# The result's way out of a token and channel mixing kernel: VectorE 32x32 transposes and small stores in place of TensorE transposes, token down begun on half of h1, a second bank for early attention values

## The chip, the cores and the metric

The kernel runs on one core of one Trainium2 chip. The metric is the device time of one execution in microseconds; the median of several executions counts, lower is better. All matrix work is fp32 in quality: most products are made from two fp32r parts of each operand (hi and lo), three matmuls for each product.

## The reference

Three stages, batch B = 4, sequence S = 576, model width DM = 512.

```python
attn = softmax(mask(q @ k.T / 8)) @ v      # 8 heads of 64; window 32, for heads 4 to 7 dilated by 4
x = attn as [B, S, 512]
# feed forward with token shift
xk = mu_k * x + (1 - mu_k) * x_prev;  xr = mu_r * x + (1 - mu_r) * x_prev
x = sigmoid(xr @ w_r) * (relu(xk @ w_k) ** 2 @ w_v)              # w_k 512x1024, w_v 1024x512
# token and channel mixing
h = relu(x.T @ w_tok1) @ w_tok2            # 576 -> 256 -> 576 over the tokens
u = x + h.T
out = u + relu(u @ w_ch1) @ w_ch2          # 512 -> 1536 -> 512
```

## The kernel before, in words

The program has no loops at run time. Each stage is a list of steps, and a step is a small set of functions, one for each engine that takes part; every engine's instruction stream is its functions in the order of the list. Engines meet at semaphores only, so the order of the list is the order on each engine's queue, and a waiting instruction holds all that is behind it on its engine.

Phase 1 holds attention and the feed-forward stage. Attention works in 24 groups n (12 blocks of 192 tokens, each for the plain heads and for the dilated ones). The first four groups run in a prologue whose list is written out by hand (`prologue`): transposes of q and k into the two halves of the PSUM tensor `tq2`, scores into `s2`, softmax over VectorE, GpSimd and ScalarE, transposes of p, then `weighted_values(n)` (L605) into the bank `o_ps`, from which `x_evict(n)` (L621) copies into X on ScalarE. `weighted_values(n)` waits until group n - 1's copy is done, since there is one such bank. `keep_warm` steps put idle matmuls between. Behind the copy of group 3 the feed-forward stage begins: `difference` (L645, GpSimd, its subtraction L651), `mix` (L654, VectorE, L664), and the first products of `up` (L744). From then on attention groups 4 to 23 are strewn between the feed-forward units. X holds the transposed activations (features on partitions, tokens along the row).

Phase 2 (`phase2_body`) takes one batch b after the other:

- `x_transpose` (L971) transposes the batch's activations `xcur` (loaded by a GpSimd request, `load_x` L936) into rows, and splits them; these steps of batch b + 1 are in the list of batch b, between the last channel-up tile and the last two channel-down tiles.
- `token_up` (L1006), two tiles m of 128x512 of h1: 15 matmuls each (5 token tiles x 3), then Relu into the high part on ScalarE (L1025) and the low part on VectorE (L1029).
- `out_transpose` (L1144), five tiles of 120 (the last 96) tokens: four TensorE transposes each of U into one of the four work banks (L1153), a ScalarE copy into an `ost` buffer (L1159), and one store of up to 120 rows of 2 KB by SyncE (L1163).
- `token_down` (L1032), eight tiles (half h of the tokens, feature tile d): 6 matmuls each, and U = product + xcur on VectorE (L1050). In batch 0 alone the four tiles of the first half are made by `first_token_down` (L1053), which starts on the first 128 rows of h1 and needs the second later.
- `token_parts` (L1069) splits u; `channel_up` (L1084) makes 24 tiles of 12 matmuls, each with a Relu (L1103) and a low part (L1107); `channel_down` (L1110) follows two tiles behind and adds into four accumulators `acc[d]`, 12 matmuls for each f (L1131 to L1133), with one signal `c2_done` at the end of the four.
- `finish` (L1135) adds the four accumulators into U on VectorE (L1141), once for each half h, after the last channel-down of the half.

Products with two parts go through `product` (L686), whose three matmuls are L694, L695 and L696. The four work banks (`bank[0]`, `bank[1]`, the halves of `tq2`) are used in turn in the order of the table `ORDER`: 8 token-down tiles, 24 channel-up tiles, 5 of x, 2 of token-up, 5 output tiles, 44 in all, a multiple of 4. `work_free` makes TensorE wait until the user four places earlier has been read. The list of a batch ends like this:

```python
            return steps + ups + [out_transpose(b, tt) for tt in range(NTT)]
```

so TensorE's order at a batch boundary is: token up of the next batch, the 20 transposes of this batch's result, token down of the next.

## Time and profile before

| | us |
|---|---|
| median of 3 executions | 768.98 (768.02 to 769.06) |
| the profiled execution | 766.38 |
| its span on the core | 764.5 |
| TensorE matmuls busy | 737.9 (97%) |
| VectorE busy | 354.7 (46%) |
| ScalarE busy | 257.3 (34%) |
| GpSimd busy | 221.2 (29%) |

The span runs from the first to the last recorded instruction of the profiled execution; the execution's own time is 1.9 us longer. Matmuls overlap: a matmul of 128x288 is shown with some 0.3 us, but the next one starts 0.13 us after it. So the distance between starts is the cost in a row of matmuls, and the shown duration counts only where something waits for the last one. A bracket at the end of a timeline row gives the idle time of the engine before the row and who ended it.

### The profile page before, as it was taken

The numbers are of one execution on the slowest core, as the hardware profiler recorded it, in microseconds if no ns is written. First come the engines' busy times: TensorE is split into PE (matmuls) and PEld (weight loads), VectorE is DVE, ScalarE is ACT, GpSimd is POOL, SyncE is SP. The second block draws the span as 40 slices with busy tenths as digits, with TensorE's granted clock in tenths as the row PEclk, the third lists the DMA queues.
The fourth block names the chain that finished last, engine by engine and source line by source line (L and its number), as shares of the span: only waits on it lengthen the run. The fifth ranks groups of instructions, "written<-read, shape, count | busy, mean of one in ns | idle before, by whom it ended". The sixth has DMA issues, their size and how long they took to land.

```text
span 764.5 us, 15730 instructions
## 1 busy us (share of the span) xinstructions
PE 737.9 (97%) x6650; PEld 712.8 (93%) x6650; DVE 354.7 (46%) x590; ACT 257.3 (34%) x641; POOL 221.2 (29%) x237
## 2 busy tenths in 40 slices
PE   7889899999999999999999999999999999999997
PEld 7778899898998989899989999999999999999997
DVE  6488756676575757666661213412134121341211
ACT  4565453535345353525351112411124111241112
POOL 5395664546456464636018000000000000000000
PEclk9999999999999999999999999999999999999999
DMA  9922132120230230020641000300003000020002
GB/s 199 289 50 66 22 78 59 28 61 23 55 75 21 52 76 19 1 63 1 235 158 42 21 1 1 124 3 1 1 1 124 1 1 1 1 63 1 2 1 63
DMA packets 67942, 39.82 MB, mean 52 GB/s; under 512 B 55264, under 2 KB 59168, under 8 KB 67872
## 3 DMA queue, kind: packets, MB, share of 16 engines
q1 hardware_dynamic: 62559, 33.30, 17.0%
q0 software_dynamic: 1088, 4.72, 1.8%
q10 hardware_dynamic: 4224, 0.79, 0.7%
q8 instruction: 53, 0.87, 0.5%
q14 instruction: 18, 0.14, 0.1%
HBM read 29.36 MB, written 4.72 MB: 45 GB/s over the span
## 4 chain that ended last, share of the span: by engine, by line
PE 84%; POOL 6%; issue 3%; ACT 3%; DVE 3%; ACTq 1%; DVEq 0%; POOLq 0%
PE bank L694 14%; PE bank L695 13%; PE bank L696 13%; PE tq L694 5%; PE tq L696 5%; PE tq L695 5%; PE s L1133 3%; PE bank L1133 3%; PE bank L1132 3%; PE bank L1131 3%; PE s L1131 3%; PE s L1132 3%; PE bank L615 3%; PE bank L587 2%; PE s L497 2%
## 5 line engine op out<-in xcount | busy, mean ns | idle before, releaser
L694 PE MATMUL bank<-k_hi,WV_hi 128*128 128x288 f32 x256 | 79.1, 309 | 0.0
L694 PE MATMUL bank<-xk_hi,WK_hi 128*128 128x288 f32 x224 | 69.5, 310 | 9.6 <-DVE kr L757 8.4
L695 PE MATMUL bank<-k_hi,WV_lo 128*128 128x288 f32 x256 | 76.3, 298 | 0.0
L696 PE MATMUL bank<-k_lo,WV_hi 128*128 128x288 f32 x256 | 76.0, 297 | 0.0
L1107 DVE SCALAR_TENSOR_TENSOR h_lo<-tq,h_hi 128x288 fp32r<-128x288 f32 x48 | 22.0, 458 | 115.9 <-ACT h_hi L1103 115.9
L1107 DVE SCALAR_TENSOR_TENSOR h_lo<-bank,h_hi 128x288 fp32r<-128x288 f32 x48 | 22.0, 458 | 115.5 <-ACT h_hi L1103 115.5
L772 POOL TENSOR_TENSOR k_lo<-kr,k_hi 128x288 fp32r<-128x288 f32 x64 | 53.4, 836 | 71.8 <-ACT k_hi L768 71.5
L695 PE MATMUL bank<-xk_hi,WK_lo 128*128 128x288 f32 x224 | 66.2, 296 | 0.0
L696 PE MATMUL bank<-xk_lo,WK_hi 128*128 128x288 f32 x224 | 66.0, 294 | 0.0
L805 DVE RECIPROCAL rg<-rg 128x288 f32<-128x288 f32 x32 | 62.5, 1953 | 1.1
L1103 ACT ACTIVATE h_hi<-tq 128x288 fp32r<-128x288 f32 x48 | 19.7, 411 | 127.2 <-PE tq L696 127.2
L1103 ACT ACTIVATE h_hi<-bank 128x288 fp32r<-128x288 f32 x48 | 19.7, 410 | 117.8 <-PE bank L696 117.8
L1133 PE MATMUL s<-h_lo,C_hi 128*128 128x288 f32 x192 | 57.0, 297 | 0.0
L1133 PE MATMUL bank<-h_lo,C_hi 128*128 128x288 f32 x192 | 57.0, 297 | 0.0
L1132 PE MATMUL bank<-h_hi,C_lo 128*128 128x288 f32 x192 | 56.9, 297 | 0.0
L941 POOL DMA_DIRECT2D xcur<-X x4 | 3.2, 798 | 185.8 <-DVE U L1050 168.6
L1131 PE MATMUL s<-h_hi,C_hi 128*128 128x288 f32 x192 | 56.9, 297 | 0.0
L1131 PE MATMUL bank<-h_hi,C_hi 128*128 128x288 f32 x192 | 56.9, 296 | 0.0
L1132 PE MATMUL s<-h_hi,C_lo 128*128 128x288 f32 x192 | 56.7, 295 | 0.0
L694 PE MATMUL bank<-u_hi,C_hi 128*128 128x288 f32 x192 | 56.7, 295 | 0.0
L694 PE MATMUL tq<-u_hi,C_hi 128*128 128x288 f32 x192 | 56.7, 295 | 0.0
L695 PE MATMUL bank<-u_hi,C_lo 128*128 128x288 f32 x192 | 56.7, 295 | 0.0
(155 smaller groups left out, 2172.4 us busy)
## 6 DMA issues: line engine op xcount, KB each, us to landing
C_raw<-in_moe_w_ch SPq DMA_DIRECT2D x6, 1024.0 KB, 11.6
xcur<-X POOLq DMA_DIRECT2D x4, 1152.0 KB, 5.8
qraw<-in_q SPq DMA_DIRECT2D x20, 192.0 KB, 3.5
kraw<-in_k SPq DMA_DIRECT2D x20, 192.0 KB, 4.0
out_x<-ost SPq DMA_DIRECT2D x16, 240.0 KB, 2.7
vt<-in_v SPq DMA_DIRECT2D x40, 80.0 KB, 2.5
vt<-in_v SPq DMA_DIRECT2D x7, 320.0 KB, 3.3
WK_raw<-in_moe_w_k SPq DMA_DIRECT2D x4, 512.0 KB, 7.9
```

The source lines that it names most:

```text
L497: last = e.matmul(s2[64 * a:64 * a + 64, c0:c0 + KB], qT[rows, 256 * s + 64 * c:256 * s + 64 * (c + 1)], keys(rows, s, c), start=True, sto ...
L615: last = e.matmul(o_ps[64 * h:64 * h + 64, SU * s + QB * c:SU * s + QB * (c + 1)], raw_v(n, slice(0, KB), 2 * s + h)[:, D * c:D * (c + 1)] ...
L694: e.matmul(out_ap, wh, xh, start=start and i == 0, stop=False)
L695: e.matmul(out_ap, wl, xh, start=False, stop=False)
L696: last = e.matmul(out_ap, wh, xl, start=False, stop=stop and i == len(kts) - 1)
L772: e.tensor_tensor(lo, t, hi.bitcast(F32), ALU.subtract).then_inc(Z.lo_done, 1)
L805: e.reciprocal(t, t).then_inc(Z.r_done, 1)
L1103: e.activation(hi, ps, ACT.Relu).then_inc(Z.h2h_done, 1)
L1107: e.scalar_tensor_tensor(lo, ps, 0.0, hi.bitcast(F32), ALU.max, ALU.subtract).then_inc(Z.h2l_done, 1)
L1131: e.matmul(o_, wh, xh, start=f == 0, stop=False)
L1132: e.matmul(o_, wl, xh, start=False, stop=False)
L1133: return e.matmul(o_, wh, xl, start=False, stop=f == FT2 - 1)
```

## The change

It has five parts.

1. *Result of the batches.* The `out_transpose` steps are gone. `finish` is now four steps, one for each feature tile d, each waiting for its own tile's last matmul only; for that, `channel_down` signals `c2_done` after each of the four tiles (four times for each f), and waits on it count by four. `out_blocks(b, h, d)` transposes the 128x288 piece of U on VectorE in blocks of 32x32 into `blocks[h]`. For the first half of the tokens (h = 0) these steps stand in the channel loop of the second half, behind channel-down tiles 1 to 4; for h = 1 (batches 0 to 2) they stand behind the last `finish`, ahead of token up. `store(b, h)` issues 16 requests on SyncE, for each d and each group of 32 partitions one: 288 pieces of 32 values (128 bytes) each.
2. *Last half of the last batch.* `last_transposes(d)` makes three TensorE transposes of 96 tokens as soon as feature tile d is finished; `last_rows(g)` copies two feature tiles at a time (ScalarE two thirds, VectorE one third) and SyncE stores them in one request of 288 pieces of 1 KB.
3. *Token down.* `first_token_down` now serves every batch. h1's second tile gets its low part in two pieces of 256 columns, each with its own signal, and token down waits for the first piece before the feature tiles 0 and 1 of kt = 1 and for the second before tile 2.
4. *Work banks.* The output tiles are no longer in `ORDER`: 39 users for a batch, so the bank of a user now depends on the batch too.
5. *Early values.* Groups 1 and 3 of attention put their values into the upper half of `tq2` in place of `o_ps`; so groups 1, 2 and 3 wait for the copy of the group two before. The transposes of group 4's keys, which use the same half, wait for the copy of group 3.

The core of the diff:

```diff
-        ost = [at(f"ost{i}", [P, DM], F32, 4 * DM * i) for i in range(4)] + [at("ost4", [P, DM], F32, o)]
-        assert NTT == 5 and 4 * DM <= XB
-        o += 4 * DM
+        blocks = [at(f"blocks{h}", [P, DT * HALF], F32, 4 * DT * HALF * h) for h in range(2)]
+        rows3 = at("rows3", [P, 3 * DM], F32, -(-4 * XB // 64) * 64)
...
+                    if n == 4 and g == 1:
+                        e.wait_ge(Z.x_done, 4)
...
+        def o_bank(n):
+
+            return tq2[:, 512:1024] if n in (1, 3) else o_ps
...
             def tensor(e):
                 e.wait_ge(Z.ptb_done, n + 1)
                 e.wait_ge(*v_landed(n))
-                wait(e, Z.x_done, n)
+                if n in (1, 3):
+                    e.wait_ge(Z.k_done, 4)
+                wait(e, Z.x_done, n - 1 if n in (1, 2, 3) else n)
...
-                [("x", i) for i in range(NTT)] + [("t1", i) for i in range(2)] + [("ot", i) for i in range(NTT)]
+                [("x", i) for i in range(NTT)] + [("t1", i) for i in range(2)]
         TB = len(ORDER)
-        READ = {"x": (Z.xtl_done, NTT, 1), "t1": (Z.h1l_done, 2, 1), "t2": (Z.u_done, 8, 0), "c1": (Z.h2l_done, 2 * FT2, 0),
-                "ot": (Z.os_done, NTT, 0)}
-        assert TB % 4 == 0
-
-        def work_bank(kind, i):
-            return work[ORDER.index((kind, i)) % 4]
+        READ = {"x": (Z.xtl_done, NTT, 1), "t1": (Z.h1l_done, 3, 1), "t2": (Z.u_done, 8, 0), "c1": (Z.h2l_done, 2 * FT2, 0)}
+
+        def work_bank(b, kind, i):
+            return work[(TB * b + ORDER.index((kind, i))) % 4]
...
+            pieces = [(0, DM)] if m == 0 else [(0, DM // 2), (DM // 2, DM)]
+
+            def part(t, c):
+                return t[:, DM * m + c[0]:DM * m + c[1]]
...
-            def vector(e):
-                e.wait_ge(Z.h1h_done, n + 1)
-                e.scalar_tensor_tensor(lo, ps[:, :], 0.0, hi.bitcast(F32), ALU.max, ALU.subtract).then_inc(Z.h1l_done, 1)
+                e.activation(part(h1[0], (0, DM)), ps[:, :], ACT.Relu).then_inc(Z.h1h_done, 1)
+
+            def vector(e):
+                e.wait_ge(Z.h1h_done, 2 * b + m + 1)
+                for c in pieces:
+                    e.scalar_tensor_tensor(part(h1[1], c), ps[:, c[0]:c[1]], 0.0, part(h1[0], c).bitcast(F32), ALU.max,
+                                           ALU.subtract).then_inc(Z.h1l_done, 1)
...
-        def first_token_down():
-
-            def tensor(e):
-                e.wait_ge(Z.x2_done, DT * NU)
-                e.wait_ge(Z.h1l_done, 1)
+            return dict(tensor=tensor, vector=vector) if h else dict(vector=vector)
+
+        def first_token_down(b):
+
+            def tensor(e):
+                if b == 0:
+                    e.wait_ge(Z.x2_done, DT * NU)
+                e.wait_ge(Z.h1l_done, 3 * b + 1)
                 for d, kt in ((0, 0), (1, 0), (2, 0), (0, 1), (1, 1), (2, 1), (3, 0), (3, 1)):
                     if kt == 0:
-                        work_free(e, 0, "t2", d)
-                    elif d == 0:
-                        e.wait_ge(Z.h1l_done, 2)
-                    last = product(e, work_bank("t2", d)[:, 0:HALF], h1, cols(DM, P * d, P), T2, cols(S, 0, HALF), [kt],
+                        work_free(e, b, "t2", d)
+                    elif d in (0, 2):
+                        e.wait_ge(Z.h1l_done, 3 * b + (3 if d else 2))
+                    last = product(e, work_bank(b, "t2", d)[:, 0:HALF], h1, cols(DM, P * d, P), T2, cols(S, 0, HALF), [kt],
                                    start=kt == 0, stop=kt == 1)
                     if kt == 1:
                         last.then_inc(Z.t2p_done, 1)
...
-                    e.wait_ge(Z.c2_done, n - NH2 + 1)
+                    e.wait_ge(Z.c2_done, DT * (n - NH2 + 1))
...
-                    last = channel_product(e, d, f, i % NH2)
-                last.then_inc(Z.c2_done, 1)
+                    channel_product(e, d, f, i % NH2).then_inc(Z.c2_done, 1)
...
-        def finish(b, h):
-            def vector(e):
-                e.wait_ge(Z.c2_done, 2 * FT2 * b + FT2 * (h + 1))
+        def finish(b, h, d):
+            c = slice(S * d + HALF * h, S * d + HALF * (h + 1))
+
+            def vector(e):
+                e.wait_ge(Z.c2_done, DT * (2 * FT2 * b + FT2 * (h + 1) - 1) + d + 1)
                 e.wait_ge(Z.uh_done, 8 * b + 8)
+                e.tensor_tensor(U[:, c], acc[d][:, 0:HALF], U[:, c], ALU.add).then_inc(Z.fin_done, 1)
+            return dict(vector=vector)
+
+        out_done = (Z.out_done0, Z.out_done1)
+        OUT = 16 * 4 * DT
+
+        def out_blocks(b, h, d):
+
+            def vector(e):
+                e.wait_ge(Z.fin_done, 8 * b + 4 * h + d + 1)
+                if d == 0:
+                    wait(e, out_done[h], OUT * b)
+                e.transpose(blocks[h][:, HALF * d:HALF * (d + 1)], U[:, S * d + HALF * h:S * d + HALF * (h + 1)])\
+                    .then_inc(Z.ob_done, 1)
+            return dict(vector=vector)
+
+        def store(b, h):
+
+            def sync(e):
                 for d in range(DT):
-                    c = slice(S * d + HALF * h, S * d + HALF * (h + 1))
-                    e.tensor_tensor(U[:, c], acc[d][:, 0:HALF], U[:, c], ALU.add).then_inc(Z.fin_done, 1)
-            return dict(vector=vector)
-
-        def out_transpose(b, tt):
-            n = NTT * b + tt
-            nt = rows_of(tt)
-            ps = work_bank("ot", tt)
-
-            def tensor(e):
-                work_free(e, b, "ot", tt)
-                e.wait_ge(Z.fin_done, 8 * b + (4 if TT * tt + nt <= HALF else 8))
-                for d in range(DT):
-                    last = e.transpose(ps[0:nt, P * d:P * (d + 1)], U[:, S * d + TT * tt:S * d + TT * tt + nt], ident[:, :])
-                last.then_inc(Z.otp_done, 1)
-
-            def scalar(e):
-                e.wait_ge(Z.otp_done, NTT * b + tt + 1)
-                e.wait_ge(Z.ost_free, b + 1)
-                e.activation(ost[tt][0:nt, :], ps[0:nt, :], ACT.Copy).then_inc(Z.os_done, 1)
+                    e.wait_ge(Z.ob_done, 8 * b + 4 * h + d + 1)
+                    for g in range(4):
+                        c0 = P * d + 32 * g
+                        e.dma_start(out[b, HALF * h:HALF * (h + 1), c0:c0 + 32].rearrange("(c i) n -> i c n", i=32),
+                                    blocks[h][32 * g:32 * (g + 1), HALF * d:HALF * (d + 1)].rearrange("p (c n) -> p c n", n=32))\
+                            .then_inc(out_done[h], 16)
+            return dict(sync=sync)
+
+        TL = HALF // 3
+
+        def last_transposes(d):
+
+            def tensor(e):
+                if d == 0:
+                    e.wait_ge(Z.h2l_done, 2 * FT2 * B)
+                e.wait_ge(Z.fin_done, 8 * B - DT + d + 1)
+                for t in range(3):
+                    c0 = 2 * P * (t % 2) + P * (d % 2)
+                    last = e.transpose(work[2 * (d // 2) + t // 2][0:TL, c0:c0 + P],
+                                       U[:, S * d + HALF + TL * t:S * d + HALF + TL * (t + 1)], ident[:, :])
+                last.then_inc(Z.lt_done, 1)
+            return dict(tensor=tensor)
+
+        def last_rows(g):
+
+            dst = tiles(rows3[0:TL, :], 3)[:, :, 2 * P * g:2 * P * (g + 1)]
+
+            def scalar(e):
+                e.wait_ge(Z.lt_done, 2 * g + 2)
+                e.activation(dst[:, 0:2], tiles(work[2 * g][0:TL, :], 2), ACT.Copy).then_inc(Z.ra_done, 1)
+
+            def vector(e):
+                e.wait_ge(Z.lt_done, 2 * g + 2)
+                e.tensor_copy(dst[:, 2], work[2 * g + 1][0:TL, 0:2 * P]).then_inc(Z.rv_done, 1)
 
             def sync(e):
-                e.wait_ge(Z.os_done, n + 1 + NTT)
-                e.dma_start(out[bass.ds(b, 1), TT * tt:TT * tt + nt, :].rearrange("b t n -> (b t) n"), ost[tt][0:nt, :])\
-                    .then_inc(Z.out_done, 16)
-                if tt == NTT - 1:
-                    e.wait_ge(Z.out_done, 16 * (n + 1))
-                    e.sem_inc(Z.ost_free, 1)
-            return dict(tensor=tensor, scalar=scalar, sync=sync)
+                e.wait_ge(Z.ra_done, g + 1)
+                e.wait_ge(Z.rv_done, g + 1)
+                e.dma_start(out[B - 1, HALF:S, 2 * P * g:2 * P * (g + 1)].rearrange("(t p) n -> p t n", p=TL), dst)\
+                    .then_inc(out_done[1], 16)
+            return dict(scalar=scalar, vector=vector, sync=sync)
...
-                    if seq[i - 2][1] == FT2 - 1:
-                        steps.append(finish(b, seq[i - 2][0]))
-            return steps + ups + [out_transpose(b, tt) for tt in range(NTT)]
+                    h, f = seq[i - 2]
+                    if h == 1 and 1 <= f <= DT:
+                        steps.append(out_blocks(b, 0, f - 1))
+                    if f < FT2 - 1:
+                        continue
+                    steps += [finish(b, h, d) for d in range(DT)]
+                    if h == 1 and not last:
+                        steps += [out_blocks(b, 1, d) for d in range(DT)]
+            if last:
+                return steps + [store(b, 0)] + [last_transposes(d) for d in range(DT)] + [last_rows(g) for g in range(2)]
+            return steps + [store(b, 0), store(b, 1)] + ups + [first_token_down(nxt)]
```

## Rows read from the trace of the kernel before

**Rows 1.** The page, part 1: busy time, share of the span, instructions.

```profile
PE 737.9 (97%) x6650; PEld 712.8 (93%) x6650; DVE 354.7 (46%) x590; ACT 257.3 (34%) x641; POOL 221.2 (29%) x237
```

**Rows 2.** Windows: length, then PE, PEld, DVE, ACT, POOL busy; granted clock, DMA share, GB/s.

```profile
82.00:84.00 2.00, 2.00 (x10) 2.00 (x9) 1.97 (x4) 0.88 (x3) 1.06 (x2) 0.50 0.03 8
84.00:86.00 2.00, 2.00 (x35) 1.73 (x36) 0.55 (x2) 0.76 (x2) 1.21 (x1) 0.74 0.00 0
...
400.00:500.00 100.00, 99.80 (x736) 98.05 (x735) 26.14 (x58) 20.63 (x46) 18.04 (x10) 1.00 0.12 36
```

**Rows 3.** Timeline at the end of batch 0: start, duration, engine, line, what.

```profile
475.93 0.81 DVE L1141 TENSOR_TENSOR U<-bank,U 128x288 f32<-128x288 f32 x2
...
481.62 0.40 PE L696 MATMUL tq<-xT_lo,T_hi 96*128 96x512 f32 x1
481.86 0.60 PE L1153 MATMUL tq<-ident,U 128*120 128x128 f32 x4
...
482.69 0.69 DVE L1029 SCALAR_TENSOR_TENSOR h_lo<-tq,h_hi 128x512 fp32r<-128x512 f32 x1 [2.73 <-ACT h_hi L1025]
...
484.28 0.38 PE L694 MATMUL bank<-T_hi,h_hi 128*128 128x288 f32 x1
484.49 0.30 PE L695 MATMUL bank<-T_hi,h_lo 128*128 128x288 f32 x1
```

**Rows 4.** Timeline of TensorE in token down and in channel up of batch 1.

```profile
484.76 0.29 PE L694 MATMUL bank<-T_hi,h_hi 128*128 128x288 f32 x1
...
490.72 0.30 PE L694 MATMUL bank<-u_hi,C_hi 128*128 128x288 f32 x1
...
497.08 0.29 PE L694 MATMUL tq<-u_hi,C_hi 128*128 128x288 f32 x1
...
498.53 0.29 PE L696 MATMUL tq<-u_lo,C_hi 128*128 128x288 f32 x1
```

**Rows 5.** Timeline of batch 0's first token down.

```profile
390.31 0.40 PE L694 MATMUL bank<-T_hi,h_hi 128*128 128x288 f32 x1 [0.22 <-DVE h_lo L1029]
...
392.07 0.82 DVE L1050 TENSOR_TENSOR U<-bank,xcur 128x288 f32<-128x288 f32 x2 [1.82 <-DMA xcur<-X]
...
392.59 0.40 PE L694 MATMUL bank<-T_hi,h_hi 128*128 128x288 f32 x1
```

**Rows 6.** Timeline of the end of the program.

```profile
757.34 0.82 DVE L1141 TENSOR_TENSOR U<-s,U 128x288 f32<-128x288 f32 x2 [3.89 <-PE bank L1133]
...
759.04 0.62 PE L1153 MATMUL bank<-ident,U 128*120 128x128 f32 x4 [0.86 <-DVE U L1141]
...
760.67 0.59 ACT L1159 ACTIVATE ost<-tq 96x512 f32<-96x512 f32 x1
760.81 0.80 SPq L1163 DMA_DIRECT2D out_x<-ost  x2
```

**Rows 7.** Timeline of the prologue's end, attention groups 2 and 3.

```profile
28.38 1.14 PE L615 MATMUL bank<-pT,X 80*64 80x48 f32 x32 [0.73 <-ACT X L632]
...
29.55 0.88 ACT L632 ACTIVATE X<-bank 128x192 f32<-128x192 f32 x2 [1.32 <-PE bank L615]
...
30.51 1.29 POOL L651 TENSOR_TENSOR dif<-X 128x288 f32<-128x288 f32 x2 [0.91 <-ACT X L632]
...
32.17 1.24 PE L744 MATMUL bank<-x,WK_raw 128*128 128x288 f32 x4 [0.59 <-DVE x L664]
```

**Rows 8.** Costliest groups on VectorE of shape 128x288: busy, mean ns, idle before.

```profile
L805 DVE RECIPROCAL rg<-rg 128x288 f32<-128x288 f32 x32 | 62.5, 1953 | 1.1
...
L1141 DVE TENSOR_TENSOR U<-s,U 128x288 f32<-128x288 f32 x16 | 6.6, 454 | 11.3 <-PE bank L1133 11.3
```

**Rows 9.** Requests: size and landing; issue times on SyncE in ns; two in a timeline.

```profile
out_x<-ost SPq DMA_DIRECT2D x16, 240.0 KB, 2.7
...
L429 SPq DMA_DIRECT2D X<-in_v x8: 432/443/447, 10.8 to 14.2; - x8
...
18.78 6.24 SPq L365 DMA_DIRECT2D kraw<-in_k  x2
```

More of the change, by code:

```diff
@@ L961, in work_free @@
                 b, before = b - 1, before + TB
[L962 to L963 removed]
             k, n = ORDER[before]
             s, per, ahead = READ[k]
[L966 removed]
+            n = 2 * n if k == "t1" else n
+            wait(e, s, per * (b + ahead) + n + 1)
         def rows_of(tt):
```

34 lines of the change are left out of this document (12 added, 22 removed).

## The prediction

> **What bounds the kernel now.** I read the page's busy times first, then the windows by stage, then the timeline where the stages meet, at the start and at the end. TensorE is busy 97% of the span [rows 1]; in a stretch of the last stage it is busy 99.8 of 100 us at full granted clock, with VectorE and ScalarE at a quarter or less [rows 2]. There, work taken off TensorE shortens the time one for one, and work put on VectorE costs nothing until TensorE comes to wait for it. The timeline at the end of batch 0 shows what stands between two batches: the last token-up matmul of the next batch, twenty transposes of the result (20 more at each of the two later boundaries, placed the same), and only then token down [rows 3]. At the end and in the prologue TensorE isn't the limit, so there I follow the chain.
>
> **Boundaries, three times.** The transposes begin at 481.86 and token down at 484.28: 2.42 us, and the first matmul after them takes 0.21 us to the next one instead of 0.13 [rows 3]; so 0.08 more for a restart. After the change the nine matmuls that need only the first half of h1 begin at 481.86 and last 9 x 0.13 = 1.19, to 483.05. The tenth needs the low part of the second half. VectorE starts it at 482.69 and takes 0.69 for 512 columns; it is now cut in two. From 0.69 for 512 and 0.45 for 288 [rows 3, 8] a straight line gives 0.42 for 256, so the first piece ends at 483.11 and TensorE goes on at about 483.15: a wait of 0.10 and a restart of 0.08. The second piece ends by 483.5 and its reader starts at 483.9. Gain per boundary 2.42 + 0.08 - 0.10 - 0.08 = 2.32, three times 7.0. Bounds 2.1 (the cut pieces each as slow as a 288-column operation and a late start) to 2.5 (no wait at all): 6.3 to 7.5.
>
> **VectorE's transposes** aren't in the trace. Eight of 128x288 come to each of the three batches, four in the last. Four stand among the channel loop, where VectorE works a quarter of the time, and are free at any price below some 2 us (24 matmuls at 0.13, 3.2 us, for each of them). The other four stand at the boundary, after the final additions, which end at about 475.93 + 0.81 = 476.7 today, and ahead of h1's low parts. The first low part must be there at 481.86, and takes 0.69: so 481.1 - 476.7 = 4.4 us are free, 1.1 each; more, as the additions now start tile by tile. The nearest row is an addition of the same shape at 0.45; the far bound is the reciprocal at 1.95 [rows 8]. I take 0.45, which costs nothing. Below it nothing can be gained either: cover.
>
> **Signals.** channel_down now signals after each of its four tiles, 3 x 96 = 288 signals more. Token down has eight signals among the 45 intervals from 484.76 to 490.72, 0.1324 each; channel up has none in the 11 from 497.08 to 498.53, 0.1318 each [rows 4]. The difference over 45 intervals is 0.03 us, for eight signals 4 ns each, within the reading's 0.01; with that at most 9 ns. I take 0, with up to 2.6 us in the range. The Trainium skill, "TensorE: Matmul & The Clock Gate", section "The cost: per-tile semaphore tail", says that increments on completions queue up at 26.3 ns each. By that figure the 288 would cost an estimated 7.6 us and leave little of the gain; it is fitted on packed tiles, and no run here shows it.
>
> **First token down (batch 0).** It already starts on half of h1. The cut piece would end 0.27 earlier at the wait before 390.31; but the matmul at 392.59 waits for an addition that waits for xcur's transfer (1.82 us, to 392.07) [rows 5], and that transfer does not move. Gain 0.
>
> **The end.** Today the four additions start together at 757.34, the transposes that need them at 759.04, the last copy runs 760.67 to 761.26, the last store is issued right behind it and the span ends at 764.50 [rows 6]: 3.24 after the copy. After: each tile's addition starts when its own three matmuls are done; the first three hide under the last matmuls, the fourth runs 757.34 to 757.79. Twelve transposes of 96 rows at 0.12 (2.42 for twenty [rows 3]) run from about 757.1, one interval behind the last matmul; the last three start at 758.2, their result is there at 758.7 (two more and a last one of 0.3), the copy of 512 columns ends at 759.4 (0.59 and a step of 0.05). Plus 3.24 is 762.6. The last store carries 288 KB instead of 192; 240 KB land in 2.7 us [rows 9], less than the 3.24 for a larger one than today's last, so bytes are the small part and I add an estimated 0.3: 762.9, gain 1.6. If all of the 3.24 grew with the bytes, the gain would be 0.3; if nothing did and the copies of the two halves ran quicker, 2.5. The four VectorE transposes and sixteen stores of the first half start about 30 us before the end and lie under the channel loop.
>
> **Prologue.** Group 3's values wait 0.73 us for the copy of group 2's out of the same bank; then come the copy, the differences, the mixing and the matmul at 32.17 [rows 7]. With a second bank this chain moves up by 0.73; GpSimd has by then finished the two differences before it. Group 1's bank saves nothing: its matmuls waited for p, not for the bank. The new wait on group 3's keys and the transposes of group 4 are long met. I take 0.7. Bounds: 0, if GpSimd's queue, which the chain runs through from 37 us on, gives it back; and 1.5 more or less from the clock. That is because after two waits near 80 us the granted clock stood at 0.50 (the 1.2 GHz level) for 2 us and at 0.74 for 2 more [rows 2]: 1.0 + 0.5 lost, which another alignment may save or double.
>
> **Stores.** Each batch issues 32 requests of 288 pieces of 128 bytes in place of 5. SyncE takes 0.44 us for a small load request; the worst pair in the trace took 6.24 for two, with much in flight [rows 9]. Only SyncE is behind them; 32 x 0.44 = 14 us against a batch of 95. Cost 0.
>
> **Sum.** 7.0 + 1.6 + 0.7 = 9.3 on a span of 764.5, whose execution took 766.38: to 757.1. The median shown is 768.98, 2.6 above that execution, and the change touches nothing that explains the 2.6; so 759.7.
>
> **The rivals.**
> 1. *Signals cost.* With 9 ns each 2.6 us, 762.3; within my range. Only against [rows 4] could it be more: the signals would have to cost more in channel_down than they do in token down, and at three times the 9 ns the gain would still not be gone (767.5). Chance 0.06, of which 0.02 for more than 9 ns.
> 2. *VectorE becomes late at the boundary.* Transposes at the reciprocal's 1.95: the additions end about 475.6, then 7.8 us, so h1's first low part ends at 484.1 and token down starts there, as today. The 7.0 goes, 766.6 remains. Against it: of the costliest groups on VectorE with this shape only the reciprocal is above 0.5. The price begins to count between 1.1 and 1.4 each. Chance 0.04.
> 3. *The stores back up (slower).* The last batch's first half can be stored from about 719.3 on (19 groups of twelve matmuls at 0.1324 before 757.1 is 727, less the 7.7 gained by then), sixteen requests; the result's last stores stand behind them on SyncE. With t each, they hold the end from 719.3 + 16t + 3.2 > 755, t > 2.0, and make it slower than before from t > 2.6. At the worst pair's 3.12 the span ends at 772.4, the median is at 777. For it: pieces of 128 bytes. Against it: 0.44 for small requests in a row [rows 9]. The Trainium skill, "DMA: Bandwidth & Descriptors", section "Specifications", says that transfers under 512 B are read, modified and written; no run here has such a store. Chance 0.04.
> 4. *The bank and the tail give nothing, or the clock falls once more*: 7.0 - 1.5 + 0.5 = 6.0 or so, 763.0. Chance 0.08.
>
> **Chances.** Forecast 0.78, the four rivals 0.22. The forecast's own low end, with the clock's 1.5 back or a tail of 2.5 with boundaries of 2.5, is some 2.7 below: 757.0. The high end is 763.0 and holds rival 4 and rival 1 up to 9 ns; rivals 2 and 3 and the rest of 1 stay out. A measurement of this kernel can tell 0.2%, 1.5 us, from no change. All but rivals 2 and 3 are faster; rival 2 is faster by 0.3% at its price and nothing if dearer: same 0.03, slower 0.04, faster 0.93.
>
> **What would show it.** Right: at the boundary token down's matmuls directly behind token up's, with one wait of 0.1 to 0.2 for h1's low part; VectorE transposes of 0.3 to 0.6 us; matmul intervals of 0.13 in channel_down; group 3's values without a wait; 5 to 5.7 us from the last channel matmul to the end. Wrong: intervals above 0.14 behind channel_down's tiles (rival 1), TensorE waiting more than 1 us for h1 at the boundary (2), SyncE's store requests at over 2 us each (3), a second stretch at clock 0.5 (4).

## The result, and the profile after

| us | before | after |
|---|---|---|
| median beside each other, 4 executions each | 769.02 (768.02 to 772.4) | 761.85 (760.34 to 763.75) |
| the profiled execution | 766.38 | 763.75 |
| its span | 764.5 | 761.9 |
| first feed-forward matmul of the prologue starts at | 30.44 | 37.13 |
| from there to the first token-up matmul | 351.40 | 351.21 |
| first token-up matmul to the end of the span | 382.66 | 373.58 |

The ratio after to before is 0.990, interval 0.9861 to 0.994: 7.2 us less, where 9.3 was forecast. Executions of this kernel differ by some us, and the table's last three rows say where. The third stage repeats to within 0.5 us: 373.4 to 373.8 in the seven profiles in which it is as in the changed kernel, 382.5 to 382.9 in the four in which it is as before. The prologue doesn't repeat. So nearly every reading below splits the span at those two matmuls. The profiled pair differs by 2.6 only: 9.08 gained in the third stage, 0.19 in the middle, and 6.69 lost in the prologue. Two executions of a kernel below took 1014 and 1185 us, at a mean granted clock of 0.65 and 0.56; the ratios leave them out.

The page of the changed kernel; the first line answers to [rows 1], the store line to [rows 9]. The digits are the granted TensorE clock in 40 slices of 19 us.

```profile
PE 733.7 (96%) x6582; PEld 708.6 (93%) x6582; DVE 365.6 (48%) x624; ACT 248.5 (33%) x623; POOL 221.5 (29%) x237
...
PEclk8899999999999999999999999999999999999999
...
out_x<-blocks SPq DMA_DIRECT2D x112, 36.0 KB, 1.7
```

TensorE has 68 matmuls less: 80 transposes out, 12 in. VectorE has 11 us more and is no nearer its limit. The first two slices of the clock, 9 in the kernel before, are 8, so TensorE ran slower for part of the first 38 us.

**The boundary.** Timeline at the end of batch 0, where [rows 3] show the kernel before (bracket: idle time before the row and who ended it).

```profile
481.08 0.85 DVE L1148 TENSOR_TENSOR U<-bank,U 128x288 f32<-128x288 f32 x2
...
481.27 0.40 PE L703 MATMUL bank<-xT_hi,T_hi 120*128 120x512 f32 x1
...
481.85 1.54 DVE L1160 STREAM_TRANSPOSE blocks<-U 128x288 f32<-128x288 f32 x4
...
485.54 0.69 DVE L1038 SCALAR_TENSOR_TENSOR h_lo<-bank,h_hi 128x512 fp32r<-128x512 f32 x1 [2.15 <-ACT h_hi L1033]
...
487.90 0.40 PE L705 MATMUL tq<-xT_lo,T_hi 96*128 96x512 f32 x1
...
488.14 0.30 PE L703 MATMUL tq<-T_hi,h_hi 128*128 128x288 f32 x1
...
488.96 0.76 DVE L1038 SCALAR_TENSOR_TENSOR h_lo<-tq,h_hi 128x256 fp32r<-128x256 f32 x2 [2.74 <-ACT h_hi L1033]
...
489.20 0.29 PE L705 MATMUL bank<-T_lo,h_hi 128*128 128x288 f32 x1
...
489.45 0.40 PE L703 MATMUL tq<-T_hi,h_hi 128*128 128x288 f32 x1
...
494.71 0.30 PE L703 MATMUL tq<-u_hi,C_hi 128*128 128x288 f32 x1
```

The reader is to see three things. Token down follows token up after 0.24, one interval of a 512-column matmul (487.90, 488.14). Nine matmuls later the next starts 0.25 after its neighbour instead of 0.13: the one small wait, for h1's first low piece. And VectorE's four transposes take 1.54 together and end at 483.39; VectorE then idles 2.15 us until h1's first tile is there for its low part (485.54), so they delay nothing. SyncE's 16 requests start at 482.34 and take 9.79. From the first token-up matmul of a batch to its first channel-up it is 494.71 - 481.27 = 13.44 us; before it was 490.72 [rows 4] - 474.99 = 15.73. The row of the kernel before that this starts from:

```profile
474.99 0.40 PE L694 MATMUL bank<-xT_hi,T_hi 120*128 120x512 f32 x1
```

The later boundaries give 13.44 and 13.46 against 15.76 and 15.73.

**The end.** Timeline of the last us, against [rows 6].

```profile
755.30 0.86 DVE L1148 TENSOR_TENSOR U<-s,U 128x288 f32<-128x288 f32 x2 [2.66 <-PE s L1140]
...
756.12 0.86 DVE L1148 TENSOR_TENSOR U<-bank,U 128x288 f32<-128x288 f32 x2
756.18 0.30 PE L1140 MATMUL bank<-h_lo,C_hi 128*128 128x288 f32 x1
...
756.32 0.82 PE L1186 MATMUL bank<-ident,U 128*96 128x128 f32 x6
...
757.79 0.97 SPq L1206 DMA_DIRECT2D out_x<-rows  x2
...
757.83 0.59 ACT L1197 ACTIVATE rows<-tq 96x512 f32<-96x512 f32 x1
```

The additions now start while TensorE is still in the last channel matmuls, and the transposes follow at one interval. From the last channel matmul (756.18) to the end of the span (761.9) it is 5.72; before it was 7.49 (757.01 to 764.5). The last channel matmul of the kernel before:

```profile
757.01 0.30 PE L1133 MATMUL bank<-h_lo,C_hi 128*128 128x288 f32 x1
```

**VectorE's transposes and the stores**, grouped by the tile `blocks` (columns: duration in ns as least, median, most; first and last start).

```profile
L1171 SPq DMA_DIRECT2D out_x<-blocks x112: 315/455/1952, 450.1 to 738.5; - x112
L1160 DVE STREAM_TRANSPOSE blocks<-U x28: 434/467/469, 449.6 to 736.6; 128x288 f32<-128x288 f32 x28
...
DMA to landing us min/median/max: 1.5/1.7/3.3
```

**The start.** Timeline of the first 9 us of the changed kernel. SPq and ACTq are the requests issued by SyncE and ScalarE.

```profile
0.74 1.93 SPq L364 DMA_DIRECT2D qraw<-in_q  x4
...
4.32 1.78 ACTq L891 DMA_DIRECT2D mus<-in_moe_mu_k  x1
...
4.53 3.01 SPq L428 DMA_DIRECT2D vt<-in_v  x4
...
6.13 1.61 ACTq L891 DMA_DIRECT2D mus<-in_moe_mu_r  x1
...
7.85 0.49 ACT L466 ACTIVATE qT<-tq 128x384 f32<-128x384 f32 x1 [4.62 <-issue]
...
8.87 1.35 PE L498 MATMUL s<-kT,qT 64*64 64x80 f32 x32 [3.08 <-ACT kT L474]
```

The same stretch of the kernel before:

```profile
0.88 1.93 SPq L365 DMA_DIRECT2D qraw<-in_q  x4
...
4.53 4.08 SPq L429 DMA_DIRECT2D vt<-in_v  x4
...
5.62 1.28 ACTq L882 DMA_DIRECT2D mus<-in_moe_mu_r  x1
...
7.01 0.49 ACT L465 ACTIVATE qT<-tq 128x384 f32<-128x384 f32 x1 [3.83 <-issue]
...
8.03 0.78 PE L497 MATMUL s<-kT,qT 64*64 64x80 f32 x32 [1.50 <-ACT kT L473]
```

In the changed kernel SyncE's first request is 0.14 earlier, its `vt` requests are quicker, ScalarE's requests end at 7.74 instead of 6.90. ScalarE's first copy comes 0.84 later, TensorE waits 3.08 for it instead of 1.50, and the 32 score matmuls of the group, already at the lower clock, take 1.35 instead of 0.78. Windows of the changed kernel (length, busy time of PE, PEld, DVE, ACT, POOL, granted clock, DMA share, GB/s) show what follows:

```profile
8.00:12.00 4.00, 3.13 (x43) 2.99 (x44) 1.62 (x2) 1.49 (x4) 0.00 (x0) 0.53 1.39 175
12.00:16.00 4.00, 4.00 (x51) 3.61 (x51) 2.06 (x4) 1.24 (x3) 1.56 (x2) 0.61 1.07 295
...
24.00:28.00 4.00, 4.00 (x50) 3.72 (x52) 0.89 (x2) 2.22 (x7) 1.26 (x1) 0.67 1.04 221
28.00:32.00 4.00, 4.00 (x38) 3.88 (x35) 0.43 (x3) 1.54 (x5) 1.25 (x1) 0.50 1.17 274
```

The granted clock falls to 0.50, the 1.2 GHz level, at 8.3, while TensorE still waits, and comes back at 15.1. It falls again from 25.3 to 32.2, behind a wait of 1.74 us that ends at 23.95. The profile names this wait "issue": it shows nothing that TensorE waited for. In the kernel before all of 0 to 40 us ran at 1.00.

### The profile page after: what moved, and what is told of

It is laid out like the page before. It is cut to its first block, busy times and chain, and to the rows that moved or that the text cites. A ratio compares the mean times of both kernels' runs of the same rounds, so it can differ in the third digit from the quotient of the medians.

```text
span 761.9 us, 15692 instructions
## 1 busy us (share of the span) xinstructions
PE 733.7 (96%) x6582; PEld 708.6 (93%) x6582; DVE 365.6 (48%) x624; ACT 248.5 (33%) x623; POOL 221.5 (29%) x237
## 4 chain that ended last, share of the span: by engine, by line
PE 83%; POOL 6%; issue 3%; DVE 3%; ACT 2%; DMA 1%; ACTq 1%; DVEq 0%; POOLq 0%
PE bank L703 14%; PE bank L704 13%; PE bank L705 13%; PE tq L703 4%; PE tq L705 4%; PE tq L704 4%; PE bank L1140 3%; PE bank L1139 3%; PE s L1140 3%; PE bank L1138 3%; PE s L1138 3%; PE s L1139 3%; PE bank L624 3%; PE bank L588 2%; PE s L498 2%
## 5 line engine op out<-in xcount | busy, mean ns | idle before, releaser
L704 PE MATMUL tq<-u_hi,C_lo 128*128 128x288 f32 x192 | 56.6, 295 | 0.0
```

The lines of the kernel that those rows point to most:

```text
L704: e.matmul(out_ap, wl, xh, start=False, stop=False)
```

## The experiments

Where a ratio is given it is to the kernel before on the same chip, with its interval. "Third stage" is the stretch from the first token-up matmul to the end of the span, of the profiled execution.

### The changed kernel again, beside the next three

> The changed kernel itself, once more, as the yardstick for this chip. Theory: its gain from the first token-up matmul to the end is fixed by the schedule (9.1 us: three boundaries of 2.3 to 2.45 and 1.8 at the end), and what varies from run to run lies ahead of 45 us, where the granted clock falls to 0.50 after TensorE has waited for ScalarE's first two copies. So the ratio is 0.988 to 0.992, and the stretch from the first token-up matmul to the end of the span is within 0.2 us of 373.6 us. Rival (the small stores or the signals disturb TensorE now and then): that stretch itself varies by over 1 us.

761.83 (760.9 to 764.64, 10 executions) against 766.26 (29 executions): 0.9945, 0.9923 to 0.9967, which is outside the 0.988 to 0.992 expected. Third stage 373.58, to the hundredth the first profile's. First feed-forward matmul at 34.73, clock 0.50 for 3.4 us from 10.3 and from 24.0 again. With 29 executions of the kernel before, the gain is 4.4 us, not 7.2: the 769.0 of the first four was at the upper end of what that kernel does. The third stage gains 9.1, so something else loses some 4.7.

### One bank for early values

```diff
-            return tq2[:, 512:1024] if n in (1, 3) else o_ps
+            return o_ps
...
-                if n in (1, 3):
-                    e.wait_ge(Z.k_done, 4)
-                wait(e, Z.x_done, n - 1 if n in (1, 2, 3) else n)
+                wait(e, Z.x_done, n)
```

> The changed kernel with one bank for the early values, as before the change. Theory: group 3's value matmuls wait 0.7 us for group 2's copy again, and the first feed-forward matmul of tile 2 comes 0.7 us later behind group 2's copy; total plus 0.7 us against e1, if the clock in the prologue is the same in both. Rival (GpSimd's queue gives it back): the wait is back, but the distance from group 2's copy to GpSimd's first k_lo is within 0.2 us of e1's.

762.95, 0.9955 (0.9936 to 0.9973); first feed-forward matmul 35.11, with the same two falls of the clock. From the copy of group 2 to GpSimd's first `k_lo` it is 9.73 us with one bank (also in the kernel before) and 9.21 with two: the bank is worth 0.52 on that chain, not 0.73. GpSimd's four subtractions are next: with two banks they stand in a row without idle time and take 2.97 us (0.66 to 0.88 each, VectorE's mixing beside them), where with one bank the two pairs take 1.29 each. So the bank isn't what loses the 4.7; the prologue is as late without it.

### Token down waits for all of h1

```diff
-                e.wait_ge(Z.h1l_done, 3 * b + 1)
+                e.wait_ge(Z.h1l_done, 3 * b + 3 if b else 1)
```

> The changed kernel, but in batches 1 to 3 token down waits for all of h1's low parts before its first matmul. Theory: token down starts 1.7 us later at each of three boundaries (from 488.14 to 489.8 in the changed kernel's trace), less the wait of 0.12 and its restart that it has now: plus 1.4 to 1.6 each, plus 4.5 us in all against e1; that much of the 7.3 us from the boundaries would not have come by moving the transposes alone. Rival (VectorE's late parts could be covered otherwise): plus under 2 us.

767.69, 1.0005 (0.9977 to 1.0033), 13 executions. Third stage 377.79, so 4.21 longer. The waits of TensorE in it (total, times, longest):

```profile
PE tq L703 <- DVE h_lo L1038: 3.0, 2, 1.5
PE bank L703 <- DVE h_lo L1038: 1.5, 1, 1.5
```

One wait of 1.5 at each of three boundaries: half of h1 is worth 1.4 of the 2.3 gained at each. Taking the transposes from TensorE alone would have left 0.9, since h1's low part, hidden under them before, would be waited for.

The prologue of this profile tells something by chance. It is the lowest of the 13 executions (761.49): the clock fell once, for 3.4 us from 8.7, within a wait of 2.9, there was no "issue" wait behind 20 us, and the first feed-forward matmul starts at 30.66, 21.8 behind the first scores. Where the clock didn't fall at all (`mu` requested by GpSimd, below) it is 20.7, in the changed kernel's two profiles 28.3 and 25.6. So the first fall alone costs 1.1 us here; most of the cost is the "issue" wait and the fall behind it.

### Signals of every tile, in the kernel before

```diff
-                    last = channel_product(e, d, f, i % NH2)
-                last.then_inc(Z.c2_done, 1)
+                    channel_product(e, d, f, i % NH2).then_inc(Z.c2_done, 1)
```

with the two waits multiplied by four.

> The kernel before with one part of the change: channel_down signals after each of its four tiles, 288 signals more, and the waits count by four. Theory: nothing, within 0.3 us, in the stretch from the first token-up matmul to the end, and intervals of 0.13 us behind every tile. Rival (completion signals queue up, 26 ns each by the Trainium skill's page on TensorE, an estimate of 7.6 us): plus 7 us. By the upper bound of the reading, 9 ns each, plus 2.6 us.

765.89, 1.0003 (0.9986 to 1.002). Third stage 382.46 against 382.66: 288 signals more cost nothing that shows, less than 2 ns each by the 0.5 us to which the stage repeats. The Trainium skill, "TensorE: Matmul & The Clock Gate", section "The cost: per-tile semaphore tail", gives 26.3 ns for each; by that the stretch would be an estimated 7.6 us longer. Here, with signals 3 matmuls of 288 columns apart, the trace doesn't agree: nothing of the 7.6 shows. The tail it speaks of, increments of packed tiles at the end of a burst, wasn't tried.

### One signal for four tiles, in the changed kernel

```diff
-                    channel_product(e, d, f, i % NH2).then_inc(Z.c2_done, 1)
+                    last = channel_product(e, d, f, i % NH2)
+                last.then_inc(Z.c2_done, 1)
...
-                e.wait_ge(Z.c2_done, DT * (2 * FT2 * b + FT2 * (h + 1) - 1) + d + 1)
+                e.wait_ge(Z.c2_done, 2 * FT2 * b + FT2 * (h + 1))
```

> The changed kernel with one signal for each channel-down step instead of four, so that the four additions of a half start together after its last matmul. Theory: the last addition ends 1.1 us later, the stretch from the last channel matmul to the end of the span is 6.8 instead of 5.7 us, and the stretch from the first token-up matmul to the end 374.7 instead of 373.6; the boundaries don't change, since their additions are under cover. Rival (the signals themselves cost): the stretch gets shorter, by up to 2.6 us.

One execution, 765.86. Third stage 374.52, 0.94 longer. Its end:

```profile
757.52 0.29 PE L1141 MATMUL bank<-h_lo,C_hi 128*128 128x288 f32 x1
757.85 0.82 DVE L1149 TENSOR_TENSOR U<-s,U 128x288 f32<-128x288 f32 x2 [3.88 <-PE bank L1141]
```

The first addition starts 0.33 behind the last channel matmul, where in the changed kernel it starts 0.88 ahead of it. From the last channel matmul to the end of the span it is 6.6 against 5.7. So some 0.85 of the 1.77 at the end is the signal of each tile; by subtraction, the rest is the twelve transposes and split copies in place of twenty and whole ones, which no run takes out by itself. The time of 765.86 isn't this edit's: its clock stood at 0.50 for 10.2 us from 23.1.

### Six transposes for each one at the boundary

```diff
+                if h == 1:
+                    for j in range(5):
+                        e.transpose(blocks[h][:, HALF * d:HALF * (d + 1)], U[:, S * d + HALF * h:S * d + HALF * (h + 1)])\
+                            .then_inc(Z.ex_done, 1)
+                        e.wait_ge(Z.ex_done, 20 * b + 5 * d + j + 1)
```

> The changed kernel with each of VectorE's four transposes at a batch boundary made six times, each waiting for the one before. Theory: 24 transposes of about 0.46 us take 11 us from 481.85; the cover ends 0.69 us before token down's start at 488.14, that is after 5.6 us; so each boundary grows by 5 to 5.8 us, the stretch from the first token-up matmul to the end from 373.6 to 389 to 391 us, and TensorE waits for h1's low part at the start of token down. Rival (cover smaller, since VectorE's later work stands behind too): more than 391.

One execution, 784.42; third stage 397.0, 23.4 longer. The waits, and the boundary's timeline:

```profile
PE tq L703 <- DVE h_lo L1038: 12.0, 2, 6.0
PE bank L703 <- DVE h_lo L1038: 6.0, 1, 6.0
```

```profile
491.44 0.61 PE L703 MATMUL tq<-T_hi,h_hi 128*128 128x288 f32 x1 [5.97 <-DVE h_lo L1038]
```

That is more than the 389 to 391 expected. Once VectorE is late, TensorE waits for it: 18.0 in three waits. The other 5.4, 1.8 a boundary, go with the clock: it stands at 0.50 for 6.8 us around each wait, at the first from 487.8, within the wait, to 494.6, 3.1 us behind its end. The mechanism of rival 2 is real; it wants transposes of more than a us each, and they take 0.39 to 0.47.

### The two increments put back

What else stood in the prologue? The changed kernel no longer has `ost_free` and `os_done`, and with them fell two semaphore increments that SyncE executed ahead of its first request. This puts two increments of unused semaphores in their place:

```diff
+            e.sem_inc(Z.du_done, 1)
+            e.sem_inc(Z.dv_done, NTT)
```

> The changed kernel with two semaphore increments on SyncE ahead of its first request, on semaphores that nobody reads: the kernel before had two such increments there, and the change deleted them with the old result buffers. Theory: without them SyncE's requests start at 0.74 us instead of 0.88, share the issue path otherwise with ScalarE's, and ScalarE's requests for mu end 0.4 to 1.1 us later; TensorE then waits over 1.9 us for the first copies and its clock falls to 0.50 near 9 us. With them put back, the first request is at 0.88 again, ScalarE's first copy at 6.6 to 7.0, no fall of the clock before 20 us, the first feed-forward matmul at 28 to 31 us instead of 34.7, and the median 4 to 5 us under e1's (757). Rival (the layout of code or memory, or chance): the first copy stays at 7.4 to 8.1 and the median within 1 us of e1's 761.8.

756.75 (754.26 to 760.01, 6 executions), 0.9865 (0.9842 to 0.9888). Two instructions more, 5 us less, though on another chip than the 761.83; the two ratios' intervals are apart. Its start:

```profile
0.88 1.93 SPq L364 DMA_DIRECT2D qraw<-in_q  x4
...
4.53 4.05 SPq L428 DMA_DIRECT2D vt<-in_v  x4
...
7.20 0.49 ACT L466 ACTIVATE qT<-tq 128x384 f32<-128x384 f32 x1 [4.01 <-issue]
...
8.22 1.34 PE L498 MATMUL s<-kT,qT 64*64 64x80 f32 x32 [1.69 <-ACT kT L474]
...
11.87 1.11 PEld L498 LDWEIGHTS s<-kT,qT 64*64 64x64 f32 x32 [0.22 <-issue]
...
15.92 0.62 PEld L498 LDWEIGHTS s<-kT,qT 64*64 64x64 f32 x32
```

SyncE's first request is back at 0.88, its four `vt` requests take 4.05 (3.01 without), ScalarE's copy is at 7.20 (7.85), the wait is 1.69 (3.08), and there is no "issue" wait behind 20 us. The first feed-forward matmul starts at 31.06, the third stage is 373.57.

The granted clock needs care here. The view shows 1.00 over all of 0 to 40 us, but this trace has no record of the clock ahead of 13.9 us, and a stretch without records is shown as 1.00; in all other profiles the records begin at 5 to 7 us. The durations tell what happened: the 32 score matmuls at 8.22 take 1.34 us as in the changed kernel (0.78 in the kernel before), the next group's weight loads 1.11 at 11.87, and the same loads 0.62 at 15.92. So TensorE ran at the lower clock from 8.2 to near 14 us all the same. "No fall of the clock before 20 us" did not come true; what is gone is the "issue" wait and the second fall.

### The two increments taken from the kernel before

```diff
-            e.sem_inc(Z.ost_free, 1)
-            e.sem_inc(Z.os_done, NTT)
```

with the waits counted from zero.

> The kernel before without the two semaphore increments at the head of SyncE's stream (the waits on their semaphores count from zero instead), and nothing else. Theory: this alone makes the kernel before slower by 3 to 5 us (769 to 771 where the kernel before takes 766.4): SyncE's first request at 0.74, ScalarE's first copy at 7.4 to 8.1, a stretch at clock 0.50 near 9 us, the first feed-forward matmul at 33 to 36 us. Rival (the two increments only help together with something else of the old layout): within 1 us of the kernel before.

770.03 (765.9 to 774.41, 12 executions) against 767.14 (17): 1.0033, 1.0005 to 1.0062. The same edit the other way round costs 2.9 us by the medians (by the interval 0.4 to 4.8) on a kernel that is otherwise untouched. Its first request is at 0.74, the rest of its start as in the changed kernel:

```profile
6.21 1.96 ACTq L882 DMA_DIRECT2D mus<-in_moe_mu_r  x1
...
8.28 0.49 ACT L465 ACTIVATE qT<-tq 128x384 f32<-128x384 f32 x1 [5.05 <-issue]
...
9.29 0.78 PE L497 MATMUL s<-kT,qT 64*64 64x80 f32 x32 [2.76 <-ACT kT L473]
```

Clock 0.50 for 3.4 us from 10.2 and from 23.9, first feed-forward matmul at 35.16 (30.44 in the kernel before), an "issue" wait of 1.8. Everything that the changed kernel's prologue showed is there without any of its five parts. Both edits move SyncE's requests and also the place of every later instruction of SyncE; no run separates the two.

### `mu` requested by GpSimd, in the changed kernel

ScalarE's two small requests stand ahead of its first copy. This moves them to another engine's queue:

```diff
-            def scalar(e):
+            def gpsimd(e):
...
-            return dict(scalar=scalar)
+            return dict(gpsimd=gpsimd)
```

> The changed kernel with the two requests for mu issued by GpSimd instead of ScalarE, ahead of whose first copies they stand. Theory: ScalarE is free at 4 us, its first copy starts when the transposes are done, at about 5.7 us, TensorE waits under 1 us for it, the clock never falls in the prologue, and the first feed-forward matmul starts at 27.5 to 29 us: 756 us or less. Rival (the fall of the clock has another cause): a stretch at 0.50 near 10 or 24 us in spite of the early copy, median 760 or more.

755.36 (754.32 to 758.93, 5 executions), 0.9852 (0.9829 to 0.9875). Its start:

```profile
4.53 2.05 SPq L428 DMA_DIRECT2D vt<-in_v  x4
...
5.93 0.49 ACT L466 ACTIVATE qT<-tq 128x384 f32<-128x384 f32 x1 [2.71 <-PE tq L451]
...
6.95 0.78 PE L498 MATMUL s<-kT,qT 64*64 64x80 f32 x32 [0.79 <-ACT kT L474]
```

The copy now waits only for the transposes that it reads. SyncE's `vt` requests take 2.05, where in the changed kernel and its variants with `mu` on ScalarE and without the two increments they took 2.45 to 3.01; GpSimd issues `mu` from 5.42 to 7.08. First feed-forward matmul at 27.66, no stretch at 0.50 in the prologue. This holds with SyncE's first request still at 0.74: with `mu` out of ScalarE's stream the early request does no harm that shows.

### The same move in the kernel before

```diff
-            def scalar(e):
+            def gpsimd(e):
...
-            return dict(scalar=scalar)
+            return dict(gpsimd=gpsimd)
```

> The kernel before with the same move of the two mu requests to GpSimd. Theory: minus 1 to 2.5 us against the kernel before, since its prologue mostly had no fall of the clock; the difference to e7 is then the change's worth with the prologue taken out: 9.1 us from the first token-up matmul to the end, and 0.7 from the second bank. Rival: the two prologues still differ by more than 1 us.

766.52, 0.9993 (0.9975 to 1.001), 12 executions: nothing, where a gain was expected. The copy comes at 5.65, 1.36 earlier than in the profile of before, and the first feed-forward matmul at 30.78, no earlier. Timeline between:

```profile
26.79 0.32 PE L615 MATMUL bank<-pT,X 80*64 80x48 f32 x4 [1.32 <-issue]
...
27.84 1.14 PE L615 MATMUL bank<-pT,X 80*64 80x48 f32 x32 [0.73 <-ACT X L632]
```

An "issue" wait of 1.32, then the 0.73 for the bank of [rows 7], then the clock at 0.50 for 3.4 us from 28.9. What the earlier copy gave, these took back. The rival came true: the first feed-forward matmul is 3.1 us later than in the changed kernel with the same move (27.66), not 0.7. And the `vt` requests take 3.44 here without `mu` beside them on ScalarE.

### `mu` by GpSimd, one bank

```diff
-            def scalar(e):
+            def gpsimd(e):
...
-            return tq2[:, 512:1024] if n in (1, 3) else o_ps
+            return o_ps
```

with the waits of the one-bank kernel.

> The changed kernel with mu's requests on GpSimd (e7) and with one bank for the early values again: the second bank's worth with the fall of the clock near 9 us out of the way. Theory: group 3's values wait 0.7 us, the first feed-forward matmul comes 0.7 to 1.1 us later than e7's 27.66, median 756 to 756.5 against e7's 755.36. Rival (the added idle time of TensorE near 26 us makes the clock fall there more often): 1.5 to 3 us slower, with a stretch at 0.50 from 24 to 29 us.

757.95 (755.37 to 763.24), 0.9881 (0.984 to 0.9922), against 755.36 with two banks, though on another chip: 2.6 more, where the chain alone says 0.52. The profile has the "issue" wait of 1.3 and the bank's 0.74 within 3 us, as above, and the clock at 0.50 for 6.8 us from 26.8, between the two waits. The two intervals overlap, so the size is open. What the profiles of both one-bank kernels with `mu` on GpSimd do show is the pair of waits and a fall at the second or just behind it; the kernel before has the pair too (0.77 and 0.73), without a fall.

### Three idle matmuls ahead of the first scores

```diff
-                keep_warm(7), transposes(0), evictions(0), scores(0), mask_max(0), subtract_max(0),
+                keep_warm(7), transposes(0), evictions(0), keep_warm(3), scores(0), mask_max(0), subtract_max(0),
```

on top of `mu` by GpSimd. The trace shows each of them as two.

> The changed kernel with mu's requests on GpSimd (e7) and three idle matmuls on TensorE between the first transposes and the first scores, where it waits 0.8 us. Theory: the falls of the clock are out already, so nothing changes: within 0.7 us of e7. Rival: idle time there still counts, e7's slower executions (756.5 and 758.9) go, median 754.5.

755.49, 0.9841 (0.9806 to 0.9876), 5 executions from 754.71 to 755.66. The median isn't lower than without the three, the spread is 1 us instead of 4.6; with five executions each that is a hint, no more. First feed-forward matmul at 28.28, clock 1.00 in the prologue. Either of these two beats the changed kernel by 6 us and the kernel before by 11 to 12.

## Why the prediction was right, and where it was wrong

The time is inside the range, and that is in part luck: two things that the forecast left out go opposite ways. It started from the median shown, 768.98; over 29, 17 and 17 executions the kernel before has 766.3, 766.6 and 767.1. And the prologue lost some 4.7 where 0.7 was to be gained. Against 766.3 the change gains 4.4 us, less than half of the 9.3 forecast. The third stage, 8.6 of the 9.3, is right in its mechanism and its size. From 766.3 the forecast's steps give 757.0, and the changed kernel with the two increments put back has 756.75; but its prologue isn't the one forecast either (31.06 to the first feed-forward matmul, 30.44 in the kernel before), so this nearness is no proof of the 0.7.

- **Boundaries, three times 2.32: right.** 15.73 - 13.44 = 2.29, and the wait for h1's first low piece takes 0.12 more than an interval, forecast 0.18 with its restart. The later run shows how the 2.3 is made up: 1.4 of it is half of h1.
- **VectorE's transposes at 0.45: right.** 0.467, and 0.39 each in a row of four. Six times as many cost a wait of 6 us a boundary; the cover estimated at 1.1 to 1.4 each is of the right size.
- **Signals at nothing: right.** Third stage 382.46 with them, 382.66 without.
- **First token down at nothing:** 14.05 became 13.90, a gain of 0.15; the wait for the addition behind xcur (0.20 at 398.97) stayed, as forecast, and the 0.22 for h1's low part [rows 5] is gone.
- **The end, 1.6: right.** 7.49 - 5.72 = 1.77. The last copy ends at 758.42 and the span 3.48 later; the estimate for larger last stores was 3.54.
- **Stores at nothing: right, with a price near the guess.** 0.455 for a request of 128-byte pieces, as for [rows 9]; 1.95 at most, so none near the 3.12 of rival 3. SyncE's queue at the boundary is done after 9.8 us of a batch of 92.5 (481.27 to 573.77).
- **Sum of the third stage:** 3 x 2.29 + 1.77 + 0.15 = 8.8; the rest of the 9.08 is spread over the channel loops, 0.03 to 0.11 in each batch. Forecast 8.6.
- **Prologue, +0.7: wrong, and the step that failed is the list of what the change removes.** The bank itself gave 0.52 on its chain, since GpSimd, said to have finished by then, was the next to be waited for. The step priced the banks and left the start at nothing, as does the sum's "the change touches nothing that explains the 2.6". But with the semaphores `ost_free` and `os_done` went two increments at the head of SyncE's stream. The core of the diff doesn't show them, and I didn't count them, though a step's every instruction has to be. They take SyncE 0.14 us, and SyncE isn't the bound. Put back they bring 5 us, taken from the kernel before they cost 2.9. The clock's part of the range was mis-sized too: the fall near 82 us, priced at 1.5, isn't in the changed kernel's profile, and its middle stretch is only 0.19 shorter.
- **Rival 4** ("the clock falls once more", 763.0, chance 0.08) is what came nearest: 761.85 is closer to its 763.0 than to the 759.7 forecast, and there are two stretches at 0.50 that the kernel before didn't have. Its place was wrong (it thought of the waits near 80 us), and so was its reason: the bank and the tail did give something. That rival's sign, a second stretch at 0.5, is in the profile. Rivals 1, 2 and 3 are out, each with a number above.

How the prologue's loss comes about, by the fourteen profiles. The first link is shown, by two edits in opposite directions and by moving ScalarE's requests. With the increments ScalarE's first copy starts at 6.58 to 7.20 (three profiles), without them at 7.42 to 8.28 (seven), with `mu` on GpSimd at 5.65 to 6.00 (four).

The second link is an order in time that all profiles keep. Where TensorE's wait for that copy was none, 0.7, 0.8, 0.8, 1.1 and 1.5 us, TensorE kept its full clock; where it was 1.7, 1.9, 2.5, 2.6, 2.6, 2.8, 2.9 and 3.1, it ran at the lower one near 9 us (the 1.7 by its durations, as said above).

The third link, from there to the "issue" wait of 1.7 to 3.1 us near 22, holds in six of these eight; the two without it are the one with 2.9 and the one with the increments put back. From the first scores to the first feed-forward matmul it is 21.8 and 22.8 us in these two, 25.4 to 29.4 in the six, and 20.7 in the two-bank kernels without a fall. The second fall of the clock follows each of the six waits or begins within it. Shorter "issue" waits of 0.8 to 1.3 us, near 27 us, are in the kernel before and in the two with `mu` on GpSimd and one bank.

What the "issue" waits wait for isn't named by the profile, but all nine point to TensorE's instructions arriving late. The six near 22 all come after 449 recorded instructions of TensorE, the three near 27 after 705, which is 256 more. And each ends 1.3 to 1.6 us after a 16 KB packet of an instruction queue has landed. The first such packet starts at 20.3 to 21.5 us in the six, at 14.8 to 18.2 in the other eight profiles. That is my reading; no run tested it by itself. Why the packet starts late is open, and so is why ScalarE's requests end later when SyncE's start 0.14 earlier.

## What to carry to other kernels

Cost a change by its stages, each from its own fixed pair of instructions, and compare profiles by the same pairs: the third stage repeats to within 0.5 us here, while the total hides a loss of 4.7 behind a gain of 9.1. Work taken from the bounding engine is worth what the next wait leaves of it (0.9 of 2.3 here without the earlier start), so move the wait in the same edit. In a prologue, read every instruction that goes at the head of a queue, a semaphore increment too, and look at what requests on other queues it will meet. Try keeping DMA requests out of the stream of the engine whose first result the rest waits for: it brought 6 us in the changed kernel and nothing in the kernel before. And check a granted clock of 1.00 against the durations of equal instructions.

## What the runs showed of the hardware that was not expected

- A shift of 0.14 us in SyncE's first request goes with ScalarE's first copy 0.65 to 1.3 us later. SyncE's four `vt` requests take 2.5 to 3.1 us with the first request at 0.74 and ScalarE's two small `mu` requests beside them, 2.1 to 2.4 with `mu` on GpSimd; with the first request at 0.88 they take 3.5 to 4.1 and 3.4. On ScalarE the `mu` requests take 1.0 to 2.3 each. By these rows SyncE's start weighs more than `mu` beside it.
- At each of three waits of 6.0 us in the third stage the granted clock was 0.50 for 6.8 us, which cost 1.8 us beyond the wait. The waits of 1.5 us at the same place, for all of h1, brought no fall.
- All nine "issue" waits of 0.8 to 3.1 us in the prologues come after 449 or 705 recorded instructions of TensorE and end 1.3 to 1.6 us after a 16 KB packet of an instruction queue has landed.
- Four GpSimd subtractions of 128x288 fp32 in a row take 0.66 to 0.88 us each with VectorE's mixing beside them; in two pairs they take 0.66 to 0.67 each.
- A transpose of 128x288 fp32 in blocks of 32x32 takes 0.467 us on VectorE, and 0.385 each when four stand in a row: the price of an addition of the same shape.
- A store of 288 pieces of 128 bytes is issued in 0.455 us and lands in 1.7 (3.3 at most) while little else is in flight.
